# Attention scores in 64-query halves with 168 key columns, and a rearranged end of attention with the first expert layer by chunks

## What is computed

```python
# q, k, v: (4 batches, 8 heads, 768 tokens, 64); n_global = 8, n_local = 96
scores = q @ k.T / 8 + bias            # bias = -slope(head) * distance
keep = (key < n_global) | (0 <= query - key < n_local)
a = softmax(where(keep, scores, -1e9)) # per query
x = heads_joined(a @ v)                # (3072 tokens, 512)

logits = x @ phi                       # 32 slots, 4 for each of 8 experts
slot_input = softmax_over_tokens(logits).T @ x      # (32, 512)
slot_out[e] = relu(slot_input[e] @ w1[e]) @ w2[e]   # 512 -> 1024 -> 512
x = softmax_over_slots(logits) @ slot_out

out = relu(x @ w_in) ** 2 @ w_out      # 512 -> 2048 -> 512
```

## Time and profile before

| | |
|---|---|
| median of 3 runs | 539.27 us |
| time of the profiled execution | 538.73 us |
| its span, first to last instruction | 536.7 us |
| mean granted TensorE clock | 0.980 |
| PE busy | 497.5 us (93%) |
| DVE busy | 366.3 us (68%) |
| ACT busy | 345.1 us (64%) |
| POOL busy | 94.4 us (18%) |
| DMA | 77.19 MB, 144 GB/s over the span |

### The profile page before, as it was taken

One profiled execution on the slowest core, in us unless ns is written; L12 is line 12 of the kernel. 1 busy time (PEld: TensorE's weight loads), 2 busy tenths in 40 slices (PEclk: granted clock), 3 DMA queues, 4 the chain that ended last, 5 costly groups with the idle time before them and its releaser, 6 DMA issues.

```text
span 536.7 us, 12117 instructions
## 1 busy us (share of the span) xinstructions
PE 497.5 (93%) x4247; PEld 404.7 (75%) x4247; DVE 366.3 (68%) x1030; ACT 345.1 (64%) x757; POOL 94.4 (18%) x222
## 2 busy tenths in 40 slices
PE   2799989999999978878999999999999999999997
PEld 1566667766676642232478999999999999999997
DVE  5677666777667665130699897776877768777783
ACT  1778778777787730000599987766777677767750
POOL 1454444444544421230000000000000000000000
PEclk9999999999999986979999999999999999999999
DMA  6599994474544483999700101101101001011011
GB/s 246 229 401 410 398 407 155 133 272 154 187 135 137 158 308 138 376 387 386 259 1 0 41 1 41 40 0 39 39 0 39 2 37 39 0 39 39 0 40 40
DMA packets 26024, 77.19 MB, mean 144 GB/s; under 512 B 2432, under 2 KB 2432, under 8 KB 23424
## 3 DMA queue, kind: packets, MB, share of 16 engines
q1 hardware_dynamic: 21792, 64.10, 32.5%
q10 hardware_dynamic: 4192, 12.58, 6.1%
HBM read 70.39 MB, written 6.29 MB: 143 GB/s over the span
## 4 chain that ended last, share of the span: by engine, by line
PE 66%; DVE 7%; ACT 7%; DMA 6%; POOL 4%; issue 4%; SPq 4%; DVEq 0%; ACTq 0%; POOLq 0%
PE bank L1485 14%; PE bank L1484 14%; PE bank L1486 14%; ACT probs L958 6%; POOL probs L426 4%; PE bank L1456 4%; PE bank L1192 4%; PE bank L1181 4%; SPq L378 3%; DMA qkv_s<-qkv_dram 3%; DMA wo_raw<-w_out_dram 3%; PE bank L1390 2%; PE bank L1232 1%; PE bank L1207 1%; DVE probs L515 1%
## 5 line engine op out<-in xcount | busy, mean ns | idle before, releaser
L958 ACT ACTIVATE probs<-probs,nmax 128x232 f32<-128x232 f32 (+1 forms) x192 | 88.6, 463 | 52.4 <-DVE nmax L515 52.4
L426 POOL TENSOR_SCALAR probs<-probs,rden 128x232 f32<-128x232 f32 (+1 forms) x192 | 82.5, 448 | 107.6 <-DVE rden L524 107.6
L1484 PE MATMUL bank<-t_hi,s_hi 128*128 128x256 f32 x352 | 98.7, 280 | 0.0
L1485 PE MATMUL bank<-t_lo,s_hi 128*128 128x256 f32 x352 | 98.6, 280 | 0.0
L1486 PE MATMUL bank<-t_hi,s_lo 128*128 128x256 f32 x352 | 98.5, 280 | 0.0
L1066 ACT ACTIVATE g_s<-bank 128x1024 f32<-128x1024 f32 x48 | 49.0, 1023 | 30.5 <-PE bank L1456 30.5
L515 DVE CUSTOM_DVE_ANT_0 probs<-bank,bias 128x232 f32<-128x232 f32 (+1 forms) x192 | 61.6, 377 | 9.8 <-PE bank L1181 8.9
L1095 ACT ACTIVATE s_hi<-s 128x512 fp32r<-128x512 f32 x88 | 55.1, 626 | 19.1 <-DVE s L893 14.7
L1484 PEld LDWEIGHTS bank<-t_hi,s_hi 128*128 128x128 f32 x352 | 66.5, 189 | 0.0
L1485 PEld LDWEIGHTS bank<-t_lo,s_hi 128*128 128x128 f32 x352 | 66.4, 189 | 0.0
L1486 PEld LDWEIGHTS bank<-t_hi,s_lo 128*128 128x128 f32 x352 | 66.4, 189 | 0.0
(11 more groups left out here) (187 smaller groups left out, 998.0 us busy)
## 6 DMA issues: line engine op xcount, KB each, us to landing
qkv_s<-qkv_dram SPq DMA_DIRECT2D x16, 1028.0 KB, 7.1
qkv_s<-qkv_dram SPq DMA_DIRECT2D x16, 704.0 KB, 4.4
w_s<-w_dram ACTq DMA_DIRECT2D x5, 2048.0 KB, 13.4
w_s<-w_dram SPq DMA_DIRECT2D x6, 1024.0 KB, 9.7
out_dram<-o_stage SPq DMA_DIRECT2D x24, 256.0 KB, 2.0
w_a<-w_dram SPq DMA_DIRECT2D x9, 512.0 KB, 8.7
wo_raw<-w_out_dram SPq DMA_DIRECT2D x4, 1024.0 KB, 14.2
w_pre<-w_dram ACTq DMA_DIRECT2D x1, 2048.0 KB, 24.6
```

What stands on the lines that cost most here:

```text
L426: last = pool.tensor_scalar(probs[:, v % 2, m, a, 0:w], probs[:, v % 2, m, a, 0:w], rden[:, v % 2, m, a:a + 1], 1.0, ALU.mult, ALU.mult)
L958: act.activation(probs[:, v % 2, m, a, 0:w], probs[:, v % 2, m, a, 0:w], ACT.Exp, bias=nmax[:, v % 2, m, a:a + 1], scale=-1.0, accum_out=d ...
L1484: pe.matmul(OUT[n], hi, W_HI[n](at_f), start=(c == 0 and f == 0 and n in (0, 2, 4, 5)), stop=False, skip_group_check=True)
L1485: pe.matmul(OUT[n], hi, W_LO[n](at_f), start=False, stop=False, skip_group_check=True)
```

## The change

1. **Scores.** A wide tile's product of 128 queries by 232 columns becomes two of 64 queries by 168 columns (L1204 of the changed kernel). The host puts the keys in another order: 64 of the 96 earlier keys, the 8 global ones, the remaining 160. Queries 0 to 63 take the first 168 of them, queries 64 to 127 the last 168. What isn't written in PSUM stays from before and falls under the mask; the first three steps of all are therefore still done whole, and so are the 128-column tiles. Bias tables, values and the iota on POOL (now two) follow the new order.
2. **End of attention.** The last logits' share goes to bank 4 and before the transposes, which go to bank 5 and are copied by ACT instead of DVE. Maxima and exponentials wait for one DVE instruction instead of three. Dispatch goes by halves of the columns (both tiles for columns 0 to 255, `den`, both for 256 to 511), and the slot sums are taken by halves. The three memsets go. Seven spare products are put between (`spare`).
3. **First expert layer.** The chunks c are outermost, the column halves inside. The next group's `w1` is loaded by chunks, four times three loads of 512 KB, each behind its chunk of `l1_0`.

```diff
@@ scores
-                        last = pe.matmul(SC[a][v % 2][:, m * KW:m * KW + w], q[rows, at_q:at_q + P], q[rows, at_k:at_k + w])
+                        if w == P or (b == 0 and v < TILES // 2):
+                            last = pe.matmul(SC[a][v % 2][:, m * KW:m * KW + w], q[rows, at_q:at_q + P], q[rows, at_k:at_k + w])
+                            continue
+                        for h in range(2):
+                            h0 = h * HALF
+                            at_s = m * KW + h * FAR
+                            last = pe.matmul(SC[a][v % 2][h0:h0 + HALF, at_s:at_s + KW - FAR],
+                                             q[rows, at_q + h0:at_q + h0 + HALF], q[rows, at_k + h * FAR:at_k + h * FAR + KW - FAR])
@@ end of attention, tensor block
+            def spare(*at):
+                for n in at:
+                    pe.matmul(bank[6][:, n * P:(n + 1) * P], ones[:, :], ident[:, :])
+            if windowed:
+                pe.wait_ge(xt_copied, BATCH * STEPS + 1)
+                mark(share(PAIRS - 1, [(STEPS - GRP + g) % 4 for g in range(GRP)], bank[4][:, 0:2 * P]), "share")
+                for m in range(2):
+                    last = pe.transpose(bank[5][:, m * P:(m + 1) * P], x_t[:, (STEPS - 1) % 4, m * P:(m + 1) * P], ident[:, :])
+                mark(last, "nat")
+                spare(0)
+                dve("log_t")
             mark(back(bank[0], log_t), "log_back")
-            pe.wait_ge(maxed, BATCH * 4)
-            mark(pe.transpose(bank[1][0:1, 0:GS], run_neg, ident[SG, SG]), "max_t")
+            spare(1)
+            pe.wait_ge(maxed, LAST * 4 + 2)
+            mark(pe.transpose(bank[1][0:1, 0:GS], new_neg, ident[SG, SG]), "max_t")
+            spare(2, 3)
...
-            mark(dispatch(bank[3], X_LAST, 0, slice(0, D)), "slot_half")
+            for t in range(2):
+                last = dispatch(bank[3][:, 0:HD], X_LAST, t, slice(0, HD))
+            mark(last, "slots_0")
...
-            mark(dispatch(bank[3], X_LAST, 1, slice(0, D)), "slot_in")
-            dve("slot_acc")
+            for t in range(2):
+                last = dispatch(bank[7][:, 0:HD], X_LAST, t, slice(HD, D))
+            mark(last, "slots_1")
+            spare(1)
+            dve("fold_n")
             for c in range(DC):
+                if c == DC // 2:
+                    dve("slot_acc_1")
                 last = pe.matmul(bank[2][:, c * SLOTS:(c + 1) * SLOTS], slot_acc[SG, c * P:(c + 1) * P], fold_n[SG, :])
@@ the first expert layer
-                for n in range(2):
-                    for c in range(DC):
+                for c in range(DC):
+                    for n in range(2):
@@ vector block
-            own(dve.memset(bank[4][:, :], 0.0), S2)
-            own(dve.memset(bank[5][:, :], 0.0), S2)
-            mark(dve.memset(bank[6][:, :], 0.0), "zero")
...
+            pe("slots_0")
+            mark(add_slots(bank[3][:, 0:HD], slice(0, HD)), "slot_acc_0")
...
-            mark(add_slots(bank[3], slice(0, D)), "slot_acc")
+            mark(add_slots(bank[7][:, 0:HD], slice(HD, D)), "slot_acc_1")
@@ scalar block
+                act.wait_ge(maxed, b * 4 + 2)
+                act.sem_inc(waits_act, 1)
+                act.activation(disp_t[SG, :], log_t[SG, :], ACT.Exp, bias=new_neg, accum_out=bat_sum).then_inc(disp_exped, 1)
                 act.wait_ge(maxed, b * 4 + 3)
                 act.sem_inc(waits_act, 1)
-                act.activation(disp_t[SG, :], log_t[SG, :], ACT.Exp, bias=new_neg, accum_out=bat_sum).then_inc(disp_exped, 1)
                 act.activation(rescale, shift, ACT.Exp).then_inc(disp_exped, 1)
@@ loads
-            for n, m in enumerate(("l1_0_half", "l1_0")):
+            for c, m in enumerate(("l1_0_0", "l1_0_1", "l1_0_2", "l1_0")):
                 sp.wait_ge(mid_pe, pe_at[m])
                 for j in range(1, 4):
-                    cols = slice(n * 512, (n + 1) * 512)
-                    sp.dma_start(w1_s[j][:, :, cols], w1_v[4 + j, :, :, cols]).then_inc((w1_in, w1_half)[n][j], 16)
+                    sp.dma_start(w1_s[j][:, c, :], w1_v[4 + j, :, c, :]).then_inc(w1_part[c], 16)
```

More of the change, by code:

```diff
@@ L38 @@
 KW = CTX + P
+HALF = P // 2
+FAR = P - HALF
 Q_AT, K_AT = 0, SEQ
@@ L235, in build @@
         w1_c_in = sem("w1_c_in")
-        w1_half = [sem(f"w1_half{j}") for j in range(4)]
+        w1_part = [sem(f"w1_part{c}") for c in range(DC)]
         w2_in = [sem(f"w2_in{j}") for j in range(4)]
@@ L264, in build @@
         out_v = out.rearrange("(t p) n -> t p n", p=P)
-        PE_M = ["log_back", "max_t", "disp_back", "max_b", "slot_half", "den", "slot_in", "si_t",
-                "l1_0_half", "l1_0", "ht_0", "l2_0", "st_0", "parts_0", "parts_1", "parts_2", "parts_3",
-                "l1_1_half", "l1_1", "ht_1", "l2_1", "st_1", "mix", "m0", "m1", "m2", "m3"]
-        ACT_M = ["weight", "relu_0", "relu_1", "mix_gh"]
-        DVE_M = ["max_row", "disp", "neg_diff", "zero", "w_sum", "fold_n", "slot_acc", "si_t", "comb_rec",
+        PE_M = ["share", "nat"] * windowed + ["log_back", "max_t", "disp_back", "max_b", "slots_0", "den", "slots_1", "si_t",
+                "l1_0_0", "l1_0_1", "l1_0_2", "l1_0", "ht_0", "l2_0", "st_0", "parts_0", "parts_1", "parts_2", "parts_3",
+                "l1_1_0", "l1_1_1", "l1_1_2", "l1_1", "ht_1", "l2_1", "st_1", "mix", "m0", "m1", "m2", "m3"]
+        ACT_M = ["x_nat"] * windowed + ["weight", "relu_0", "relu_1", "mix_gh"]
+        DVE_M = ["log_t"] * windowed + ["max_row", "disp", "neg_diff", "w_sum", "slot_acc_0", "fold_n", "slot_acc_1", "si_t", "comb_rec",
                  "relu_0", "h_t_0", "so_0", "so_t_0", "comb_t_0", "comb_t_1", "comb_t_2", "comb_t_3",
@@ L555, in add_share @@
                     return dve.tensor_copy(log_t[SG, :], SHARE[SG, :])
-                return dve.tensor_tensor(log_t[SG, :], log_t[SG, :], SHARE[SG, :], ALU.add)
+                return dve.tensor_tensor(log_t[SG, :], log_t[SG, :], part[SG, :], ALU.add)
             def copy_logits(b, back):
@@ L608, in _ @@
                         step(b, s, True)
-                for s in range(STEPS, STEPS + 4):
+                for s in range(STEPS, STEPS + 3):
                     step(LAST, s, True)
@@ L688, in _ @@
             count[0] = 0
-            slot_maxima(LAST)
+            if windowed:
+                pe("share")
+                dve.wait_ge(nat_copied, BATCH * STEPS)
+                mark(add_share(LAST, PAIRS - 1, bank[4][:, 0:2 * P]), "log_t")
+                dve.wait_ge(mid_dve, dve_at["log_t"])
+            slot_maxima(LAST, windowed)
             dve.wait_ge(iotas, 6)
@@ L1030, in mark @@
                 ins.then_inc(mid_act, 1)
+            if windowed:
+                act.wait_ge(mid_pe, pe_at["nat"])
+                mark(act.activation(x_nat[:, X_LAST + TILES - 2:X_LAST + TILES, D - P:D],
+                                    bank[5][:, 0:2 * P].rearrange("p (t n) -> p t n", t=2), ACT.Copy), "x_nat")
             slot_exps(LAST)
@@ L1214, in weigh_values, with share @@
                     last.then_inc(pv_done, 1)
-            def share(p, slots):
+            def share(p, slots, to=SHARE):
                 for g in range(GRP):
-                    last = pe.matmul(SHARE[SLOTS * g:SLOTS * (g + 1), :], phi_s[:, p, :], x_t[:, slots[g], :],
+                    last = pe.matmul(to[SLOTS * g:SLOTS * (g + 1), :], phi_s[:, p, :], x_t[:, slots[g], :],
                                      tile_position=(0, SLOTS * g))
@@ L1275, in _ @@
                         step(b, s, True)
-                for s in range(STEPS, STEPS + 3):
+                for s in range(STEPS, STEPS + 2):
                     step(LAST, s, True)
@@ L1392, in _ @@
                                              tile_position=(0, 32 * j))
-                    mark(last, f"l1_{g}" + ("_half" if n == 0 else ""))
+                    mark(last, f"l1_{g}" + ("" if c == DC - 1 else f"_{c}"))
                 pe.wait_ge(mid_act, act_at[f"relu_{g}"])
```

57 lines of the change are left out of this document (35 added, 22 removed).

## The result

| | before, on the same chip | after |
|---|---|---|
| median (range, runs) | 539.39 us (538.17 to 539.53, 4) | 529.56 us (528.20 to 530.53, 4) |
| profiled execution, its span | 538.73, 536.7 us | 530.53, 528.8 us |
| mean granted clock | 0.980 | 0.990 |

The ratio of the times is 0.9822, with an interval of 0.9806 to 0.9838: faster, by some 9.6 us. The profiled execution is the slowest of the four, where before it lay 0.5 us under the median. The forecast was 530.3 us in a range of 527.5 to 535.3. The time came as forecast; of its two parts one was larger and the other, in the profiled execution, had the wrong sign.

The account below looks back on a forecast made before the run. Attention's chain ran through PE, bias, exponentials, POOL and transposes; before 80 us DMA was full. 538.73 - 0.8 (attention) - 8.0 (from there through the loads) = 529.9 us profiled, stated as 530.3 median, range 527.5 to 535.3.

Parts of the forecast that it names:

- Score blocks: Attention's score products: four tiles side by side shorten wide blocks from 0.98 to 0.71 us; first-tile blocks lengthen by 0.04.
- the issue of passes is the limit: Rival, score blocks: 55 ns a pass makes wide blocks 0.1 us longer, less shorter fill; 532 to 534 us, chance 0.06.
- one after the other: Rival, score blocks: the four tiles run singly, a wide block grows 1.5 us; 572 us in all, chance 0.04.
- two at a time: Rival, score blocks: tiles run in pairs, a wide block grows 0.3 us, cancelling the gain; 537 to 541 us, chance 0.04.
- Attention, 0.8 us: Attention after 80 us: shorter score blocks gain 0.3 us a batch over 2.6 batches; bounds 2.2 won to 0.3 lost.
- The price of 0.3 us a batch: Attention, per batch: 0.15 + 0.2 + 0.05 us won by wide blocks, 0.1 given back by first-tile blocks.
- What is won before 80 us goes into the wait for queries and keys: Early attention, DMA full: PE time saved in scores before 80 us is worth nothing.
- the clock as a rival: Rival, after attention: PE's clock still falls to half, giving 535.2 us, or 532 if only partly; chance 0.20 together.
- From x_t to the first layer, 5.0 us earlier: End of attention: first expert layer starts at 202.8 instead of 207.81 us; full clock then saves 1.9 more in it.
- Loads: First expert layer's w1 loads: flow 8.6 us earlier, ending the full DMA stretch as much earlier; the part sums to 8.0.
- PE alone gives 6.9 + 0.7 = 7.6: Last expert layer: PE's 6.9 us earlier first layer plus 0.7 us slack before the last w2 part.
- PE becomes the later of the two: After the first expert layer: DMA moves 8.6 us earlier and PE only 6.9, so PE finishes later than DMA.

Follow-up runs that it names:

- the changed kernel again: No edit: the changed kernel run and profiled a second time, on another chip; 530.00 us, ratio 0.9831.
- the loads later: Changed kernel with one w1 and one w_in load issued later in attention: 526.92 us, ratio 0.9769; the same with whole scores: 528.48 us, ratio 0.9813.
- a third load later: Changed kernel with two weight loads (w1, w_in) later, and ACT also issuing one w2 block in batch 2 instead of batch 0: 526.64 us, ratio 0.9769.
- the kernel before the last experiment: Changed kernel with two weight loads later, and 128-column first-tile score products also split into two of 64 queries: 525.25 us, ratio 0.9747.

## Why the prediction was right or wrong

**Score blocks: right.** Wide blocks 0.73 us for 0.71, first-tile blocks 0.87 for 0.86. The four tiles of 64 by 64 do run side by side; sixteen passes of 168 columns fit in 0.73 us with fill, so "the issue of passes is the limit" (up to 1.08 us) and "one after the other" (2.5) are out, and so is two at a time (1.3). The note weighed there, the Trainium skill's page TensorEngine Tiling (Array Packing), section Tiling Modes, says that changing the mode drains the engine. The trace is in line with that: first-tile blocks lose 0.05 us by the mix of forms, and keeping one form inside the block gives 0.2 back, by my estimate half of it by the form.

**Attention, 0.8 us: the size right while the clock holds, the step around it wrong.** The price of 0.3 us a batch stands: 0.8 us less (score halves alone) and 1.0 (the changed kernel again) after the landing. With the loads later, over all four batches, it is 0.95 us in the profile and 1.6 to 2.4 in the medians and ratios, for 1.2. What failed is the sentence "What is won before 80 us goes into the wait for queries and keys". It does, but I priced the longer wait at nothing. With it the clock went to half until about 85 us, and that cost 2.5 us (117.89 against 115.34), or about 1.0 in two profiles with a shorter fall. So in some runs the scores lose, and over twelve runs of the halves alone they come to nothing. I had the clock as a rival after attention only, and hadn't asked what the same effect does at the one place where the change lengthens a wait.

**From x_t to the first layer, 5.0 us earlier: right.** It is 5.4 (7.51 us after the copy, forecast 7.9). Share, dispatch and folding came nearly as worked out, dispatch halves with 1.06 for 1.0 us; the 0.4 us more is there when dispatch starts, 3.6 us after the copy where 3.9 was worked out. The clock held, 7.09 us for the layer: 1.9 as said. The rival that it falls was near: without seven small products, or with one more wait of 1.5 us, it comes true, with medians of 533.4 and 534.6 and single runs at 535 and 536, where the rival had 535.2.

**Loads: the place right, PE's part too small.** DMA moved by 9.3 and 8.3 us in two profiles, for 8.6, counted from the x_t copy to the last block of `w_out`. PE's mix moved by 8.8 and 8.3, not 7.6, and the gain of this part is 9.26 and 8.25 us for 8.0. What failed is the step "PE alone gives 6.9 + 0.7 = 7.6": it takes PE's own work between the groups as fixed. But before, the clock was at half there for some 6.8 us, from 232 to 239; in the first profile of the changed kernel it was for 3.4, and in the second never. The start of the last expert layer's `l2` shows it, before, after and again:

```profile
247.16 0.59 PE L1410 MATMUL bank<-w_s,h_t 128*4 128x512 f32 x1 [0.58 <-DVE h_t L733]
```

```profile
240.23 0.59 PE L1461 MATMUL bank<-w_s,h_t 128*4 128x512 f32 x1 [0.58 <-DVE h_t L744]
```

```profile
235.58 0.59 PE L1461 MATMUL bank<-w_s,h_t 128*4 128x512 f32 x1 [0.57 <-DVE h_t L744]
...
242.24 0.59 PE L1461 MATMUL bank<-w_s,h_t 128*4 128x512 f32 x1 [0.69 <-DMA w_b<-w_dram]
```

Counted from the x_t copy it comes 8.2 and 9.8 us sooner, where `l2_0` had come 7.2. In the first profile PE then waits for no load in this layer; in the second it waits for three parts of `w2`, 1.7 us in all, so DMA takes back what the clock gave. "PE becomes the later of the two" is thus neither right nor wrong throughout: the last chain goes through the `w_out` load and ACT's work on it in both profiles of the changed kernel, and through PE's work in three others (without the spare products, a third load later, three memsets back). In the two profiles of the changed kernel PE is done with the mix 0.4 and 0.8 us before ACT takes it, so little parts the two, and the clock between the groups, which the sum left out, has a share in which is later.

**Sum.** In the profiled execution 1.3 us lost and 9.26 won, for 0.8 and 8.0 won: 8.0 us less by the span and 8.2 by the execution's time, 530.53 for 529.9. Two errors, 2.1 us against me and 1.3 for me, cancel in part, and how much of either a run shows hangs on where its clock falls: that the sum came out so near is partly luck. The median had 529.56 for 530.3.

## What to carry to other kernels

Ask of every wait that a change lengthens, also one that "only absorbs" the gain, what the engine's clock does after it: here such falls cost 1.0 to 2.5 us behind the wait at 78 us and 3 behind the one for `den`. A few products that fill such waits can be worth far more than they cost (some 4 us for seven at the end of attention, though no gain was shown for eight at 78 us), and weight loads that nobody needs yet should be issued behind the loads that something waits for; the second removes the wait, the first only its consequence. Where the runs of one kernel spread more than another's, look in two profiles for stretches at half clock before explaining a difference of medians.

## What the hardware showed that was not expected

- The clock falls after waits shorter than I had held possible. At 78 us it fell behind single waits of 1.58, 1.69 and 1.94 us, and after dispatch behind one of 1.54 us in the kernel with three memsets, where products of about 1 us lay on either side. In the kernel before the last experiment three waits of 1.33 us between transposes of 0.85 us were enough. In other traces like waits passed without a fall (1.50 us with the scores alone), and the changed kernel showed both behind its waits of 1.33 us between the transposes of the parts: a fall at about 228 us in one profile, none in the other. So the length of the wait alone doesn't decide, and what else does isn't shown.
- Four tiles of 64 by 64 with 32-bit data take sixteen passes of 168 columns in 0.73 us, 46 ns a pass with the fill and the change of form counted in. In the kernel with first tiles in halves, where the form before is the same, eight such passes take 0.39 us (142.39 to 142.78).
